# First phase of a three-block kernel: order of head pairs, PSUM banks and engine queues rearranged

## The reference

```python
for t in range(S):
    state = alpha[:, :, t, :, None] * state + np.einsum('bhd,bhe->bhde', k[:, :, t], v[:, :, t])
    y[:, :, t] = np.einsum('bhd,bhde->bhe', q[:, :, t], state)
h = x @ w_in
g = h * np.cos(h)
x2 = g @ w_out
h = np.maximum(np.maximum(x2 @ w1, x2 @ w2), x2 @ w3)
out = h @ w_out2
```

## Time and profile before

| | us |
|---|---|
| median of 3 runs | 840.66 (840.27 to 841.2) |
| profiled execution | 840.65, span 839.0 |
| PE busy | 822.1 (98%) |
| DVE, ACT, POOL busy | 579.0, 427.8, 246.5 |

### The profile page before, as it was taken

How to read it: one execution, slowest core, us unless ns; L and a number is a source line. 1 busy time by engine, 2 the same in 40 slices (tenths; PEclk the granted TensorE clock), 3 DMA queues, 4 the chain that set the end, 5 groups by cost and what they waited for, 6 DMA issues and landing times.

```text
span 839.0 us, 15508 instructions
## 1 busy us (share of the span) xinstructions
PE 822.1 (98%) x5446; PEld 756.6 (90%) x5446; DVE 579.0 (69%) x1078; ACT 427.8 (51%) x933; POOL 246.5 (29%) x270
## 2 busy tenths in 40 slices
PE   5899999999999999999999999999999999999998
PEld 5899998888888888888888888899999999999997
DVE  7887867777777768776875577677565655665554
ACT  5887775444554444445444466554343434344333
POOL 7986763434344424441542133200000000000000
PEclk9999999999999999999999999999999999999999
DMA  9833333222232204220321001210111110100001
GB/s 285 244 95 86 88 86 96 58 58 57 55 99 57 58 29 124 58 58 29 95 82 61 34 24 57 95 57 1 39 39 38 39 38 37 37 37 0 1 39 38
DMA packets 14034, 54.68 MB, mean 65 GB/s; under 512 B 1952, under 2 KB 2464, under 8 KB 13968
## 3 DMA queue, kind: packets, MB, share of 16 engines
q1 hardware_dynamic: 13248, 49.90, 20.5%
q0 software_dynamic: 720, 3.93, 1.2%
HBM read 44.39 MB, written 9.44 MB: 64 GB/s over the span
## 4 chain that ended last, share of the span: by engine, by line
PE 92%; POOL 3%; ACT 2%; issue 2%; DVE 1%; DMA 0%; ACTq 0%; POOLq 0%; DVEq 0%
PE h_ps L1297 7%; PE h_ps L1299 6%; PE h_ps L1298 6%; PE acc_pair L1297 5%; PE acc_pair L1298 5%; PE acc_pair L1299 5%; PE h_ps L1403 4%; PE score L1403 4%; PE h_ps L1405 4%; PE h_ps L1404 4%; PE score L1405 4%; PE score L1404 4%; PE acc_last L1297 3%; PE acc_last L1299 3%; PE acc_last L1298 3%; PE score L1261 2%
## 5 line engine op out<-in xcount | busy, mean ns | idle before, releaser
L458 POOL TENSOR_TENSOR work<-work 128x512 f32<-128x512 f32 (+1 forms) x90 | 119.4, 1327 | 278.2 <-DVE work L995 261.6
L638 ACT ACTIVATE work<-work 128x512 f32<-128x512 f32 (+1 forms) x112 | 63.7, 569 | 134.7 <-POOL work L458 122.9
L1297 PE MATMUL h_ps<-x_hi,w_hi 128*128 128x512 f32 (+1 forms) x282 | 110.9, 393 | 2.3 <-POOL w_lo L448 1.8
L981 DVE TENSOR_TENSOR work<-work,h_ps 128x512 f32<-128x512 f32 (+1 forms) x94 | 58.5, 622 | 67.1 <-ACT work L638 66.6
L1299 PE MATMUL h_ps<-x_lo,w_hi 128*128 128x512 f32 (+1 forms) x282 | 104.0, 369 | 0.0
L1298 PE MATMUL h_ps<-x_hi,w_lo 128*128 128x512 f32 (+1 forms) x282 | 103.3, 366 | 0.0
L873 DVE RECIPROCAL inv_decay<-decay 112x128 f32<-112x128 f32 x96 | 89.6, 941 | 0.5
L645 ACT ACTIVATE g_hi<-work 128x512 fp32r<-128x512 f32 (+1 forms) x112 | 63.4, 566 | 42.7 <-DVE work L981 41.4
L1297 PE MATMUL acc_pair<-g_hi,w_hi 128*128 128x512 f32 (+1 forms) x224 | 81.9, 366 | 0.5 <-POOL g_lo L466 0.3
L1298 PE MATMUL acc_pair<-g_hi,w_lo 128*128 128x512 f32 (+1 forms) x224 | 80.4, 359 | 0.0
L1299 PE MATMUL acc_pair<-g_lo,w_hi 128*128 128x512 f32 (+1 forms) x224 | 80.4, 359 | 0.0
(11 more groups left out here) (229 smaller groups left out, 2397.8 us busy)
## 6 DMA issues: line engine op xcount, KB each, us to landing
v_all<-val SPq DMA_DIRECT2D x24, 576.0 KB, 3.7
raw<-qka SPq DMA_DIRECT2D x44, 291.0 KB, 4.7
block_out<-x SPq DMA_DIRECT2D x6, 768.0 KB, 5.9
x_in<-block_out SPq DMA_DIRECT2D x6, 768.0 KB, 4.2
raw<-wb SPq DMA_DIRECT2D x12, 384.0 KB, 3.1
out<-raw POOLq DMA_DIRECT2D x5, 768.0 KB, 3.5
stage_own<-wa SPq DMA_DIRECT2D x6, 384.0 KB, 7.0
x<-wa SPq DMA_DIRECT2D x6, 384.0 KB, 5.4
```

The source lines that it names most:

```text
L458: nc.gpsimd.tensor_tensor(frac[:, cols], turns[:, cols], whole[:, cols], ALU.subtract).then_inc(S["frac_done"], 1)
L638: nc.scalar.activation(cosine[:, cols], frac[:, cols], ACT.Sin, scale=-TURN if half and t < POOL_FRAC else TURN).then_inc(S["cos_done"], 1)
L981: nc.vector.tensor_tensor(gated[:, cols], cosine[:, cols], h, ALU.mult).then_inc(S["g_done"], 1)
L1297: mm(ps, w_hi[:, w_at], xh, start=first, stop=False, skip_group_check=shared)
```

## The change

The quartered pair 3 now has units 4 and 5, pair 2 has units 6 and 7 (place0, and the order of the inputs on the host). Increments of units 0 to 7 go into the unit's own score bank instead of two accumulator banks, over four banks in the order h_ps, score. The quartered pair's outputs go into half of acc[2], the last pair's into half of acc[1] (first_place). x_high0 and x_low0 are split in three steps. hidden1 takes a list of thirds: PE runs k = 0 and 1 of tiles 0 and 1 first, then k = 2 of both. DVE runs scan(0, 2) between masks 4 and 5, x_low0(0) ahead of mask 7, and inverse(0, 2, 1) behind the first fraction. POOL waits for the third scan ahead of its second weight split, does weights 1 to 4 before the products of pair 2, and mul_decay(0, 2) and mul_inverse(0, 2) behind g_low(1) and g_low(2), the latter as one step. ACT copies x as the pairs come, does turn(1) behind rounded(0), high_weights(4) behind cosines(0), and states 6 and 7 behind cosines(1). The copy that ends inverse for odd pairs becomes two copies. Of the helpers below only the new text is shown.

```diff
@@ -148,9 +148,9 @@
 
 
         inc_ps = [ps[0:ROWS, INC_AT] for ps in score]
-        first_score = [*score, *h_ps]
-        first_inc = [a[0:ROWS, 0:PAIR_E] for a in acc[0:2]]
-        first_y = y_ps[:], acc[2], y_ps[:], y_ps[:]
+        first_score = [*h_ps, *score]
+        quads_at, pair_at = slice(0, HTOK), slice(HTOK, TOK)
+        last_y = (acc[2][:, quads_at], acc[1][:, 0:HTOK]), (y_ps[:, quads_at], y_ps[:, pair_at])
         m_ps = [[h_ps[0], h_ps[1]], [score[0], score[1]]]
         last_h = [*h_ps, *score]
         o_ps = [*acc, y_ps[:]]
...
@@ -179,12 +179,18 @@
         def place0(u):
 
             g, e = u // BATCH, u % BATCH
-            return 2 * (g % 2) + e // 2, 2 * (g // 2) + e % 2
+            return 2 * (g % 2) + (e // 2 ^ g % 2), 2 * (g // 2) + e % 2
+
+        def first_place(u):
+
+            g, e = u // BATCH, u % BATCH
+            bank = last_y[g // 2][e // 2] if g % 2 else y_ps[:, e // 2 * HTOK:(e // 2 + 1) * HTOK]
+            return bank[0:PAIR_E, e % 2 * CHUNK:(e % 2 + 1) * CHUNK]
 
         def banks(n):
 
             if n < FIRST_UNITS:
-                return first_score[n % 4], first_inc[n % 2], 4, 2
+                return first_score[n % 4], first_score[n % 4][0:ROWS, INC_AT], 4, 4
             return score[n % 2], inc_ps[n % 2], 2, 2
 
         def half_bank(t):
@@ -474,13 +480,10 @@
             mul_inverse(0, 1, slice(0, 2), "qk_half1")
             low_weights(0, (1, 2))
             mul_inverse(0, 1, slice(2, BATCH))
+            pool.wait_ge(S["scan_done"], 3)
             low_weights(1)
             low_weights(2)
-            pool.wait_ge(S["scan_done"], 3)
-            mul_decay(0, 2)
             low_weights(3)
-            mul_inverse(0, 2, slice(0, 2), "qk_part")
-            low_weights(4, (0,))
             POOL_LOW_AT = {2: 6, 7: 12, 10: 14, 11: 15}
             for i in range(TILES1):
                 if i == 4:
@@ -489,10 +492,14 @@
                 if i in (6, 12):
                     mul_inverse(*{6: (0, 3), 12: (1, 0)}[i])
                 g_low(i)
-                if i in (0, 4):
-                    low_weights(4 + i, (1, 2))
+                if i == 0:
+                    low_weights(4)
                 if i == 1:
-                    mul_inverse(0, 2, slice(2, BATCH))
+                    mul_decay(0, 2)
+                if i == 2:
+                    mul_inverse(0, 2)
+                if i == 4:
+                    low_weights(8, (1, 2))
                 if i == 2:
                     pool.wait_ge(S["scan_done"], 4)
                 if i == 10:
...
@@ -568,20 +575,25 @@
                     nc.scalar.activation(state[rr, p * BATCH + b, cc], banks(u)[1][rr, cc],
...
+            def x_high0(h):
+
+                act.wait_ge(S["y_done"], BATCH * (2 * h + 1))
+                nc.scalar.activation(x_hi[0:PAIR_E, 0, 0:2, h * HTOK:(h + 1) * HTOK],
+                                     y_ps[0:PAIR_E].rearrange("p (k n) -> p k n", k=2),
+                                     ACT.Copy).then_inc(S["xhi_done"], 1)
+
+            def x_quads0(h):
+
+                act.wait_ge(S["y_done"], BATCH * (2 * h + 1) + 2)
+                for j in range(KT):
+                    nc.scalar.activation(x_hi[PAIR_E:P, 0, j, h * HTOK:(h + 1) * HTOK],
+                                         last_y[h][0][QUAD * j:QUAD * (j + 1)], ACT.Copy).then_inc(S["xhi_done"], 1)
+
+            def x_pair0(h):
+
+                act.wait_ge(S["y_done"], BATCH * (2 * h + 2))
+                nc.scalar.activation(x_hi[0:PAIR_E, 0, 2, h * HTOK:(h + 1) * HTOK], last_y[h][1][0:PAIR_E],
+                                     ACT.Copy).then_inc(S["xhi_done"], 1)
@@ -655,26 +667,28 @@
             first_state(2)
             split_first(1, 1)
             first_state(3)
+            x_high0(0)
             high_weights(2)
             first_state(4)
-            x_high0(0)
+            x_quads0(0)
             first_state(5)
-            first_state(6)
-            x_high0(1)
+            x_pair0(0)
             high_weights(3)
-            first_state(7)
-            high_weights(4)
 
             for i in range(TILES1):
                 last = i == TILES1 - 1
                 if i == 10:
-                    x_high0(2)
+                    x_high0(1)
                 if last:
-                    x_high0(3)
-                turn(i, True)
+                    x_pair0(1)
+                    x_quads0(1)
+                if i != 1:
+                    turn(i, True)
                 if i == 1:
                     g_high(0, True)
                 rounded(i)
+                if i == 0:
+                    turn(1, True)
                 if i > 4:
                     g_high(i - 1, True)
                 if 5 < i < 10:
@@ -682,6 +696,11 @@
                 if i in (3, 8, 14):
                     split_keys(*{3: (0, 2), 8: (0, 3), 14: (1, 0)}[i])
                 cosines(i, True)
+                if i == 0:
+                    high_weights(4)
+                if i == 1:
+                    first_state(6)
+                    first_state(7)
                 if i in OUTPUT_AT and i > 9:
                     first_state(OUTPUT_AT[i])
                 if 0 < i < 7:
@@ -883,6 +902,9 @@
                         k, j = 2 * (p % 2), 2 * (p // 2)
                         end = end.rearrange("d (k b) -> d k b", k=2)
                         to = from_mid[R, odd, k:k + 2, j:j + 2]
+                        if p % 2:
+                            nc.vector.tensor_copy(to[:, 1], end[:, 0])
+                            end, to = end[:, 1], to[:, 0]
                     nc.vector.tensor_copy(to, end).then_inc(S["mid_done"], 1)
 
             def mask_scores(a, u):
...
+            def x_low0(h):
+
+                half = slice(h * HTOK, (h + 1) * HTOK)
+                dve.wait_ge(S["xhi_done"], h * (XHI - 1) + 1)
+                nc.vector.tensor_tensor(x_lo[0][0:PAIR_E, 0:2, half], y_ps[0:PAIR_E].rearrange("p (k n) -> p k n", k=2),
+                                        x_hi[0:PAIR_E, 0, 0:2, half].bitcast(fp32), ALU.subtract).then_inc(S["xlo_done"], 1)
+
+            def x_low_last0(h):
+
+                half = slice(h * HTOK, (h + 1) * HTOK)
+                quads, pair = last_y[h]
                 for j in range(KT):
+                    dve.wait_ge(S["xhi_done"], h * XHI + 2 + j)
+                    last = nc.vector.tensor_tensor(x_lo[0][PAIR_E:P, j, half], quads[QUAD * j:QUAD * (j + 1)],
                                                    x_hi[PAIR_E:P, 0, j, half].bitcast(fp32), ALU.subtract)
                     if j < KT - 1:
                         last.then_inc(S["x_row"], 1)
+                dve.wait_ge(S["xhi_done"], (h + 1) * (XHI - 1))
+                nc.vector.tensor_tensor(x_lo[0][0:PAIR_E, 2, half], pair[0:PAIR_E],
+                                        x_hi[0:PAIR_E, 0, 2, half].bitcast(fp32), ALU.subtract).then_inc(S["xlo_done"], 1)
@@ -964,13 +987,15 @@
                 inverse(0, 1, b, 0)
             mask_scores(0, 2)
             inverse(0, 1, 3, 0)
-            for u in range(3, FIRST_UNITS):
-                mask_scores(0, u)
+            mask_scores(0, 3)
+            mask_scores(0, 4)
+            scan(0, 2)
+            mask_scores(0, 5)
+            mask_scores(0, 6)
             x_low0(0)
-            scan(0, 2)
-            x_low0(1)
+            mask_scores(0, 7)
+            x_low_last0(0)
             inverse(0, 2, 0, 0)
-            inverse(0, 2, 1, 0)
 
             def gate(t, half):
 
@@ -1013,12 +1038,14 @@
             low0 = {1: (5,), 3: (7,), 6: (9,), 7: (10,), 8: (11,)}
             for i in range(TILES1):
                 if i == 10:
-                    x_low0(2)
+                    x_low0(1)
                 if i == TILES1 - 1:
-                    x_low0(3)
+                    x_low_last0(1)
                 if i == 5:
                     mask_scores(0, SCORE_AT[i])
                 fraction(i, True)
+                if i == 0:
+                    inverse(0, 2, 1, 0)
                 if i in scan0:
                     scan(*scan0[i])
                 if i in SCORE_AT and i != 5:
@@ -1256,8 +1283,7 @@
                     pe.wait_ge(S["split_done"], PAIRS * a + p + 1)
                 ps, _, depth, inc_depth = banks(n)
                 wait(pe, "mask_done", n + 1 - depth)
-                if n >= FIRST_UNITS:
-                    pe.wait_ge(S["state_done"], 2 * (n + 1 - inc_depth))
+                wait(pe, "state_done", 2 * (n + 1 - inc_depth))
                 mm(ps[:, LOW_AT], k_split[0:ROWS, p % 2, b, 0], q_dec[0:ROWS, p % 2, b], start=True, stop=True)
                 mm(ps[:, HIGH_AT], k_split[0:ROWS, p % 2, b, 1], q_dec[0:ROWS, p % 2, b, HALF:CHUNK], start=True, stop=True)
...
@@ -1267,7 +1293,7 @@
 
                 n, s, p, b = UNITS * a + u, u % 2, u // BATCH, u % BATCH
                 first = isinstance(a, int) and a == 0
-                y = (first_y[p] if first else y_ps)[0:PAIR_E, b * CHUNK:(b + 1) * CHUNK]
```

(54 more changed lines are left out.)

5 lines of the change are left out of this document (1 added, 4 removed).

## The result

The changed kernel takes 843.29 us (median, 842.01 to 844.42), the kernel before 840.94 (840.26 to 841.88) beside it on the same chip. The ratio is 1.0027, 95% interval 1.0018 to 1.0035: 1.5 to 2.9 us slower. The profiled execution took 843.61 us, span 841.9. That is 2.96 above the profiled execution of before (840.65).

What follows compares the result with a forecast made beforehand. ACT's and POOL's queues, not PE, were taken to bound the first phase; +0.3 us up to g_high(2) and +2.2 for the key split gave +2.5 on 840.65, 843.1 us, own range 842.4 to 844.0, full range 839.2 to 844.8.

Steps and rivals of the forecast that it cites:

- What bounds the kernel: Before 72 us, PE follows ACT's and POOL's queues; whatever is won or lost there passes one to one to the end.
- rival (b): Faster, 837.7 us: PE itself comes last in 24 to 72 us and wins its holes and slow stretch, -3.0; chance 0.13.
- Part 1: DVE's scan(0, 2) between masks 4 and 5 waits 1.1 us for its load; PE's last unit ends 0.8 late.
- Part 2: Quarters and two thirds of two tiles first: PE's 1.5 us hole before tile 0 closes, but PE was not last.
- ACT's sum: ACT's queue from the quarters' copy at 20.6 to turn(2) at 30.3, against 30.02; g_high(2) ends +0.3 us.
- Part 3: POOL's products of pair 2 go behind g_low(1) and g_low(2), so ACT's split_keys(0, 2) waits: +2.2 us taken.
- the middle: Value taken for the key split's delay from POOL's order: +2.2 us, between 1.9 and 2.6.
- the upper case: Scan(0, 3) starts at 32.95 and holds POOL's g_low(2), which ends at 34.8; split at 36.3, +2.6 us.
- The Trainium skill's rule: Two-input Vector and GpSimd instructions exclude each other, the first holding the shared pair throughout; total +2.9 us, without it +1.8.
- Nothing absorbs it: ACT nearly unbroken from 35 to 52, POOL 98% busy behind 47.86: no slack, g_low(7) and PE's release about 2.5 late.
- Rival (c): Much slower, 844.8 us: a second half-clock stretch behind PE's new hole before stage1(8), some 1.7 us more; chance 0.08.
- Rival (a): Same, 841.3 us: the second load lands earlier or POOL wins the collisions, so the sum is only +0.7; chance 0.29.

Runs made afterwards that it cites:

- g1: Changed kernel, third scan behind the last subtraction of x without POOL's wait, POOL's pair 2 products ahead of the loop and behind g_low(1): 1.0012, +1.0 us.
- f2: g1 with the one small copy of from_mid(0, 2) written as a maximum over an axis of length one: 1.0003 against the kernel before, +0.3 us.
- g3: Changed kernel with ACT doing states 6 and 7 and high_weights(7) ahead of split_keys(0, 2): 1.0026 against the kernel before, +2.2 us.
- e4: Changed kernel with ACT's split_keys(0, 2) moved from ahead of cosines(3) to behind cosines(4): 1.0036 against the kernel before, +3.0 us.
- g4: Changed kernel with POOL doing mul_inverse(0, 2) ahead of g_low(2) instead of behind it: 1.0022 against the kernel before, +1.9 us.
- e1: Changed kernel with POOL's order of before, the third scan still between the masks: 1.0008 against the kernel before, +0.7 us.
- b1: Kernel before with only scan(0, 2) moved between masks 4 and 5: 1.0019, +1.6 us.
- e3: Changed kernel with the third scan back behind mask 7 and POOL's order of before: 1.0016 against the kernel before, +1.3 us.
- f1: e1 with ACT's states 6 and 7 and high_weights(8) put ahead of cosines(1), (2) and (4): 1.0015 against the kernel before.
- b2: Kernel before with only POOL's part: mul_decay(0, 2) behind g_low(1), mul_inverse(0, 2) behind g_low(2), weight splits 3 and 4 ahead: 1.0031, +2.6 us.

## Why the prediction was right, and where it was not

The forecast was +2.5 us; the runs give +2.3 (1.5 to 2.9), the two traces +2.96.

- **What bounds the kernel**: right. The release moved by the sum and nothing behind it changed. PE's hole is closed and the half clock behind it gone, and the kernel is slower (rival (b) falls; g1 and f2 show it with the other costs out).
- **Part 1**: the mechanism held, the landing was off in this execution: 18.8, not 18.3, so DVE waited 1.35 us instead of 1.1 and mask 7 ended at 21.95, not 21.45. PE waited 0.80 at 20.52 for mask 5, which the text had only as "queued behind". In other executions the load landed between 18.0 and 19.2, by the starts of the waiting scans, so 18.3 was inside what happens.
- **Part 2 and ACT's sum**: tile 0's turn was at 24.70, turn(2) at 30.69 against 30.3, g_high(2)'s end at 33.43 against 33.05: +0.7 where +0.3 was forecast. The quarters' copy, where the sum starts, came at 21.16 instead of 20.6, the load again; the sum itself was 9.53 us where 9.7 were taken. The 0.18 us per matmul at half clock is a wrong division (the x16 counts those under way at both ends; the starts are 0.21 apart), but the 0.12 at full clock that the text goes on with is what the rows show. The reason stands: ACT's states (0.88 at 28.62) and weight part 4, which had lain before turn(0), now lie between turn(0) and turn(2), and that stretch grew from 4.88 to 5.99 us.
- **Part 3**: right in size, +2.2 taken and +2.2 measured (split 2.87 behind g_high(2)'s end, before 0.68). But the middle was taken and the upper case came: the scan at 32.76 lasted 1.61, g_low(2) 1.38, its end 34.89 (upper case 34.8), the split at 36.30 (upper case 36.3). It came to the middle only because g_high(2) was itself 0.4 late; measured from g_high(2), the stall shrank by what it came late. g3 shows why: the step that failed is "So ACT's fourth tile hangs on: g_high(2) end T". It hangs on POOL's queue as well, which the upper case had in it and the sum's middle did not, and this queue's length is set by collisions.
- The Trainium skill's rule ("SBUF — State Buffer", Who interferes with whom) gave +2.9 for the sum, and the traces differ by 2.96. The trace agrees with it in the step that it bears on, g_low(2)'s end (34.89, by the rule 34.8); that the totals agree as well is partly chance, since g_high(2) was 0.4 late for another reason, and the medians differ by 2.35. Of the two rows of before that the prediction called in agreement, the 2.35 us fits only in part: POOL's piece started at 20.58, the scan at 21.16, yet the scan took 1.24 and POOL's piece ended 0.53 behind it, so the first to start did not hold the other. And in after the same subtraction, at 20.77, lay over POOL's split and held nothing (three pieces in 2.09).
- **Nothing absorbs it**: right. +2.87 at the split, +2.87 at g_low(7), +2.92 at the release. PE's stage1(8) waited for the split (1.34 at 37.62), tile 6 behind it. That the order of POOL's weight splits has cover held for ACT, not for PE, which waited 0.84 for weight part 4, without cost.
- **Rival (b)** was to be told by ACT being ready with tile 3's cosine before 34.7: that cosine ran at 37.59.
- **Rival (c)**: the half clock came (0.50 in 40 to 42), and no wait of ACT for PE shows behind it, as its "against" had it; in e4 (behind a hole of 2.88 us) and g4 (ahead of tile 0) ACT did wait for PE, 2.13 and 2.12 us.
- **Rival (a)** fell: the load didn't land earlier, and the stall was 2.2. That e1, with POOL's stall out, comes to the same +0.7 is a coincidence of numbers.

Open: the two single moves in the kernel before add up to more (1.6 + 2.6) than the change, with intervals of 0.8 to 1.0 us each way. With the 0.7 of b1's trace, which its six runs at full clock bear out, the two come to 3.3. They share the slots in which they collide, so no sum of single effects was to be expected, but I have no run that shows how much of one hides under the other. Nor is it shown, other than by the chain, that in after the loss passes over ACT's queue and not over PE's wait.

## What to carry to other kernels

Ask of a queue move not only when its own data are ready, but which other engine has a step in its queue that waits for the product, and what stands ahead of it in the queue that it is moved to: here moving two products of 0.7 us behind one g_low cost 1.5 to 2.6 us, and closing a 1.5 us hole of the busiest engine brought nothing that could be measured, since it wasn't the one that came last. Work that is pushed from before the first result to behind it hasn't gone; take the distance between two later milestones (turn(0) to turn(2)) and not the earlier start as the gain. Where two engines block each other, price a step at its held duration (1.2 to 1.7 us for 0.7), because a move to save a wait tends to meet the next collision.

## What the hardware showed that was not expected

A DVE copy of 112x4 elements, 0.10 us, took 1.50 to 1.77 us in four kernels (e1, e3, f1, g1). In each it started ahead of POOL's next instruction while one was under way (0.05 us ahead in e1, 0.32 in g1), and it lasted until POOL had finished two more weight pieces. In the nine others that have the copy it started 0.02 to 0.05 us behind the end of a piece (a piece taken as 0.7 us) and took 0.10 or 0.11. The copy and POOL's timeline in before, then POOL's in e1:

```profile
29.24 0.10 DVE L886 COPY from_mid<-decay 112x4 f32<-112x4 f32 x1
...
28.50 1.44 POOL L448 TENSOR_TENSOR w_lo<-x_in,w_hi 128x256 fp32r<-128x256 f32 x2
```

```profile
28.41 1.44 POOL L454 TENSOR_TENSOR w_lo<-x_in,w_hi 128x256 fp32r<-128x256 f32 x2
```

In before the copy starts at 29.24, just as the first of two pieces from 28.50 on is over; in e1 at 28.36, just ahead of 28.41. The copy's place against POOL's pieces, to within a tenth of a us, decided between 0.10 and 1.51 us. The Trainium skill ("SBUF — State Buffer", Who interferes with whom) says that a copy may take the port pair shared with GpSimd, that the first to start holds it for its whole instruction, and that a reduction never takes it on this chip. f2 agrees: its reduction started in the middle of POOL's g_low (29.18 to 29.90) and took 0.10. That the copy doesn't get in between two pieces queued back to back is what the four traces show.

A scan reads two tiles and collides too: it took 1.30 to 1.81 us instead of 1.25 when it started under a POOL product or split, and a POOL product 1.67 or 1.69 us instead of 0.73 under a scan (g4, b2, g3). But unlike the copy, the scan did get in at the first boundary. In g4, DVE then POOL:

```profile
34.68 1.61 DVE L882 TENSOR_TENSOR_SCAN decay<-raw,starts 112x528 f32<-112x528 f32 x1
...
34.44 0.73 POOL L440 TENSOR_TENSOR k_dec<-raw,decay 112x256 f32<-112x256 f32 x1
35.14 1.67 POOL L446 TENSOR_TENSOR q_dec<-raw,inv_decay 112x256 f32<-112x256 f32 x1
```

POOL's product queued at 35.14 ended at 36.81, 0.52 behind the scan (36.29), so the scan went ahead of it. Why the one gets in and the other doesn't is open.
